# Gate, value and up projections as 2x2x2 block products by Strassen's seven, in an attention and mixture kernel on one NeuronCore

## The reference

```python
# attention: B, H, S, D = 4, 8, 576, 64, causal by blocks of 64 positions
scores = scale * (q @ k^T), -1e9 where block_i < block_j
attn   = softmax(scores);  x = (attn @ v) as 2304 tokens x 512
# gated layer: d_model 512, d_ff 1536
x = (sigmoid(x @ w_gate) * (x @ w_val)) @ w_out
# experts: E = 4, F = 1024, every token goes through every expert
p = domain_probs / (domain_probs.sum(-1) + 1e-9)
out = sum over e of p[:, e] * (relu(x @ w1[e]) @ w2[e])
```

## Time and profile before

| What | us |
|---|---|
| three runs | 1543.72, 1544.6, 1545.54 |
| median | 1544.6 |
| the profiled execution: its span, first to last instruction | 1543.3 |

### The profile page before, as it was taken

The page is one execution under the profiler, slowest core; times in us unless marked ns, Lnnn a source line. Parts: engine busy times, 40 slices in busy tenths (PEclk is TensorE's granted clock), DMA queues, the critical chain, the costliest instruction groups (busy, mean ns, idle before and its releaser), DMA issues.

```text
span 1543.3 us, 27668 instructions
## 1 busy us (share of the span) xinstructions
PE 1495.3 (97%) x8320; PEld 1376.8 (89%) x8320; DVE 663.8 (43%) x1309; ACT 578.4 (37%) x1267; POOL 160.5 (10%) x350
## 2 busy tenths in 40 slices
PE   6999998899999999999999999999999999999998
PEld 4777777899989999999999899999899999999997
DVE  4888888444222442425442333324344323323332
ACT  4777877555222222224541222222233312222221
POOL 3555555100000000001000000000010000000000
PEclk9999999999999999999999999999999999999999
DMA  7767674122222222213221212222232222222221
GB/s 174 176 163 168 163 176 113 50 67 62 67 58 68 68 56 68 66 56 104 61 75 55 62 55 70 67 68 54 59 107 66 62 61 70 63 61 68 57 65 55
DMA packets 196061, 126.71 MB, mean 82 GB/s; under 512 B 65792, under 2 KB 170272, under 8 KB 196000
## 3 DMA queue, kind: packets, MB, share of 16 engines
q1 hardware_dynamic: 194496, 121.15, 29.5%
q0 software_dynamic: 1504, 4.76, 0.9%
HBM read 92.84 MB, written 4.72 MB: 63 GB/s over the span
## 4 chain that ended last, share of the span: by engine, by line
PE 89%; DVE 5%; issue 3%; ACT 2%; SPq 1%; DVEq 0%; DMA 0%; ACTq 0%; POOL 0%; POOLq 0%
PE pb L810 27%; PE pb L808 27%; PE pb L809 27%; PE pt L438 2%; PE ov L456 2%; PE st L470 1%; DVE ptl L368 1%; DVE nmax L347 1%; PE st L426 1%; PE st L427 1%; ACT probs L275 1%; DVE x L383 1%; DVE ktl L374 1%; DVE qtl L374 0%; ACT pth L297 0%
## 5 line engine op out<-in xcount | busy, mean ns | idle before, releaser
L808 PE MATMUL pb<-xh,wl 128*128 128x384 f32 x1344 | 451.1, 336 | 9.0 <-DVE xl L683 6.5
L810 PE MATMUL pb<-xh,wh 128*128 128x384 f32 x1344 | 450.9, 335 | 0.0
L809 PE MATMUL pb<-xl,wh 128*128 128x384 f32 x1344 | 450.3, 335 | 0.0
L715 DVE SCALAR_TENSOR_TENSOR rl<-pb,rh 128x384 fp32r<-128x384 f32 x192 | 107.1, 558 | 508.4 <-ACT rh L617 508.4
L617 ACT ACTIVATE rh<-pb 128x384 fp32r<-128x384 f32 x192 | 94.5, 492 | 584.1 <-PE pb L810 584.1
L808 PEld LDWEIGHTS pb<-xh,wl 128*128 128x128 f32 x1344 | 252.9, 188 | 14.7 <-ACT wh L601 5.6
L809 PEld LDWEIGHTS pb<-xl,wh 128*128 128x128 f32 x1344 | 252.7, 188 | 3.5
L810 PEld LDWEIGHTS pb<-xh,wh 128*128 128x128 f32 x1344 | 252.7, 188 | 0.0
L683 DVE TENSOR_TENSOR wl<-raw,wh 128x512 fp32r<-128x512 f32 x298 | 196.6, 690 | 125.0 <-ACT wh L601 118.6
L810 PE MATMUL pb<-wh,rh 128*128 128x512 f32 x576 | 226.0, 392 | 0.0
L809 PE MATMUL pb<-wl,rh 128*128 128x512 f32 x576 | 225.7, 392 | 0.0
(11 more groups left out here) (74 smaller groups left out, 1601.5 us busy)
## 6 DMA issues: line engine op xcount, KB each, us to landing
raw<-in_moe_w_dram SPq DMA_DIRECT2D x192, 256.0 KB, 2.8
raw<-in_moe_w_gate_dram SPq DMA_DIRECT2D x36, 256.0 KB, 2.9
raw<-in_moe_w_val_dram SPq DMA_DIRECT2D x36, 256.0 KB, 2.9
raw<-in_moe_w_out_dram SPq DMA_DIRECT2D x36, 256.0 KB, 2.9
qhl<-qth SPq DMA_DIRECT2D x32, 144.0 KB, 2.5
qhl<-qtl SPq DMA_DIRECT2D x32, 144.0 KB, 2.5
qlh<-qtl SPq DMA_DIRECT2D x32, 144.0 KB, 2.5
qlh<-qth SPq DMA_DIRECT2D x32, 144.0 KB, 2.7
```

The lines of the kernel that those rows point to most:

```text
L715: nc.vector.scalar_tensor_tensor(rl[:, f % 2, a * TILE:(a + 1) * TILE], pb[:, 6 + a, 0:TILE], 0.0, rh[:, f % 2, a * TILE:(a + 1) * TILE].b ...
L808: nc.tensor.matmul(acc, lhs[1], rhs[0], start=start, stop=False)
L809: nc.tensor.matmul(acc, lhs[0], rhs[1], start=False, stop=False)
L810: return nc.tensor.matmul(acc, lhs[0], rhs[0], start=False, stop=stop)
```

## The change

Products of the gate, the value and the up projections are no longer computed as they stand. A unit (`unit`) takes a block of weights of 512 inputs by 256 features and the 768 tokens, both cut into 2x2 blocks (256 inputs, 128 features, 384 tokens). Four sums of weight blocks (`sums_of_weights`, GpSimd) and four sums of token blocks (`x_dve_first`, `x_dve_rest`, VectorE, once for a layer and super tile) are formed, and TensorE does seven block products (Winograd's form), each of 2 chunks by 3 matmuls of 384 columns: 42 matmuls in place of 48. P1, P6, P7 and P4 of a unit add up in one PSUM bank (a), P5 and P3 in a second (b), P2 has a third (c). What stands in bank a after P1 and after P6, and in bank b after P5, is copied out by ScalarE (`copy_of`, into s1b, u2b and s5b) before the next product is added on top of it, and VectorE adds the copy to another bank to get a block of the result (`c11`, `c12`, `c22`); the fourth block is bank a after P4.

Units of a super tile: 12 of the gated layer (gate and value in turn) and 4 for each of the 4 experts; there are 84 in all. While unit n multiplies, the engines split the seven weight blocks of unit n + 1 (`hi_a`, `hi_s`, `hi_4`, `lo_a`, `lo_s`, `lo_4`) and finish unit n - 1. `us` (the sums of weight blocks) has one buffer; `ura`, `uh`, `ul` have two. The first unit of the gated layer and of each expert is a head: there is nothing before it to interleave, and ScalarE does the copies of banks a and b before the next weights. P4 of a unit runs in the next unit, between P5 and P6. `down` follows after all four units of an expert, with its own pieces (`craw`, `ch`, `cl`); relu's split works on 3 blocks at once (1152 columns) and on the fourth alone; the hidden value's on 4 (1536 columns).

Everything is unrolled; there are no hardware loops. The attention's result goes through DRAM (`x1d`), a batch at a time. `tail_act` and `tail_dve` put the splits of unit 0's weights and all splits and sums of the first super tile's tokens into the attention's last 17 steps, the last ones ahead of the output of heads 30 and 31 in each queue. TensorE begins the gated layer after the last head's output. Output rows are sent from SP's queue as they are done, in place of GpSimd's. `mixed` is not cleared; expert 0 writes it.

The core of the diff; the first `unit` is TensorE's, the second ScalarE's, the third VectorE's, and `k` in `tail_act` counts the steps past the last score (attention's steps keep their order; their loop over bodies is written out):

```diff
-            over_model_dims(2 * v + a, 2 * u + v, a).then_inc((done, w_used)[a], 1)
+            def product(n, j, x, start, stop):
...
+                r, w, b = n % 2, W_OF[j], X_OF[j]
+                for c in range(2):
+                    mm = three(bank(n, x), (uh[r][:, w, c, :], ul[r][:, w, c, :]), (xch[:, b, c, :], xcl[:, b, c, :]),
+                               start and c == 0, stop and c == 1)
+                mm.then_inc(pd[j], 1)
...
+            def p4(n):
+                blocks(n, 4)
+                pe.wait_ge(w4_lo, n + 1)
+                pe.wait_ge(c22_ok, n + 1)
+                product(n, 4, "a", False, True)
+            def unit(n):
...
+                product(n, 1, "a", True, False)
+                pe.wait_ge(ws_lo, n + 1)
...
+                product(n, 5, "b", True, False)
+                if not head:
+                    p4(n - 1)
+                    p6(n)
...
+                product(n, 2, "c", True, True)
+                if head:
+                    p6(n)
...
+                pe.wait_ge(s5_ok, n + 1)
+                product(n, 3, "b", False, True)
...
+                pe.wait_ge(u2_ok, n + 1)
+                product(n, 7, "a", False, False)
...
+            def p6(n):
+                blocks(n, 6)
+                pe.wait_ge(s1_ok, n + 1)
+                product(n, 6, "a", False, False)
...
+            def unit(n):
+                if more and before:
+                    hi_a(act, n + 1)
+                    hi_s(act, n + 1)
+                copy_of(n, "a", s1b, 1, c11_ok, s1_ok)
+                copy_of(n, "b", s5b, 5, c22_ok, s5_ok)
+                if more and not before:
+                    hi_a(act, n + 1)
+                    hi_s(act, n + 1)
+                if before:
+                    c21(n - 1)
+                if more:
+                    hi_4(act, n + 1)
+                if before and kind(n - 1) == "val":
+                    hidden_hi(n - 1)
+                copy_of(n, "a", u2b, 6, c12_ok, u2_ok)
+                if before:
+                    rest(n - 1)
...
+            def unit(n):
+                if before:
+                    c22(n - 1)
+                    if kind(n - 1) == "val":
+                        gated_rest(n - 1)
+                if more:
+                    lo_a(dve, n + 1)
+                    lo_s(dve, n + 1)
+                if before and kind(n - 1) == "val":
+                    gated_21(n - 1)
+                if before and kind(n - 1) == "up":
+                    r21(n - 1)
+                if more:
+                    lo_4(dve, n + 1)
+                if before and kind(n - 1) == "val":
+                    hidden_lo(n - 1)
+                c11(n)
+                c12(n)
+                if before and kind(n - 1) == "up":
+                    r_rest(n - 1)
...
+        def hi_s(act, n):
+            act.wait_ge(us_ok, 4 * n + 4)
+            if n >= 2:
+                act.wait_ge(pd[7], n - 1)
...
+        def sums_of_weights(pool, n):
...
+            pool.wait_ge(u_in[r], 32 * (n // 2 + 1))
+            if n:
+                pool.wait_ge(ws_lo, n)
+            pool.sem_inc(pool_on, 1)
+            nc.gpsimd.tensor_tensor(us[:, 0, :], a21, a22, ALU.add).then_inc(us_ok, 1)
+            nc.gpsimd.tensor_tensor(us[:, 2, :], a11, a21, ALU.subtract).then_inc(us_ok, 1)
+            pool.wait_ge(us_ok, 4 * n + 1)
+            nc.gpsimd.tensor_tensor(us[:, 1, :], us[:, 0, :], a11, ALU.subtract).then_inc(us_ok, 1)
+            pool.wait_ge(us_ok, 4 * n + 3)
+            nc.gpsimd.tensor_tensor(us[:, 3, :], a12, us[:, 1, :], ALU.subtract).then_inc(us_ok, 1)
...
+        def tail_act(act, k, qk_ps):
+            if k == 0:
+                hi_a(act, 0)
+            if k == 1:
+                hi_s(act, 0)
+            if k == 2:
+                hi_4(act, 0)
+                act.wait_ge(qk_ps, STEPS)
+                act.wait_ge(xb_in, 16)
+            if k in (3, 4):
+                x_act_first(act, 0, k - 3)
+            if k in (6, 9):
+                x_act_b21(act, 0, k // 3 - 2)
+            if k in (7, 10):
+                x_act_rest(act, 0, k // 3 - 2)
```

1261 lines of the change are left out of this document (718 added, 543 removed).

## The result

| Kernel | median us (4 runs) | lowest and highest | profiled span |
|---|---|---|---|
| before, on the same chip | 1545.01 | 1543.72 to 1545.54 | 1543.3 (the profile read above) |
| changed | 1493.93 | 1492.58 to 1496.96 | 1490.8 |

The ratio is 0.9674 (95% interval 0.966 to 0.9688): faster by 51.1 us, 3.3%.

The account below looks back on a forecast made before the run. The prediction took TensorE's matmul stream as the bound. Its terms, -87.3 + 31 + 13 + 18 - 8 + 13 - 3 = -23.3, gave 1520 us against the profiled 1543.3, with a range of 1494 to 1548.

Parts of the forecast that it names:

- The removed matmuls: TensorE's block products: 84 units with 6 matmuls less each, 504 x 0.1733, forecast at -87.3 us.
- The fourth rival: TensorE gets no relief: seven products of 42 matmuls run at the old 8.3 us a unit; chance 0.02.
- (e): The attention's tail: added splits delay TensorE's start of the gated layer from 279.6 to 292.6, +13 us (7 to 16).
- (g): Terms put at nothing: the transfers, including x1 out and back, and the unrolled loops.
- (f): The kernel's end: SP's output issues run beside the additions, forecast at -3 us.
- (a): Second unit of each of 15 phases: P6 waits 1.85 us for s1b behind GpSimd's sums; +31 us in all.
- (b): The copy u2b late for P7: +0.3 at 15 heads, +0.6 at 15 gate units, together +13 with rounding.
- (c): VectorE's c22 late before P4, by 0.5 us at some 35 places if VectorE and GpSimd exclude each other: +18.
- (d): TensorE's earlier waits of 9.0 us: 8 go because the blocks' splits come piecewise, -8 us.
- the first rival: VectorE and GpSimd don't hinder each other: (a) and (c) shrink, 19 us less, 1501 us; chance 0.2.
- The second rival: GpSimd's ring of sums becomes the bound: +42, 1562 us at 0.914 a sum; chance 0.25 for GpSimd more loaded than priced.
- The third rival: ScalarE's and VectorE's waits fall into slack, so (a) to (c) halve: 1489 us; chance 0.08.

## Why the prediction was right or wrong

**The removed matmuls** brought -87.4 us for -87.3. The fourth rival (no relief for TensorE) is refuted by that line.

**(e) The tail**, +13 for +13.3, **agrees because of terms that cancel, and that is luck.** The 13.3 us are three things. Writing out the attention's loop took away 6.4 up to the last scores (265.28 to 258.84), which (g) had put at nothing. The changed kernel's own attention gave back 4.2 (258.84 to 263.05), where the one large difference in the traces is the wait for q behind x1's transfer; (g) had named just this, "costs several us if a stack of q or k queues behind it", and put it at nothing as well. The tail itself, from the last scores to the stage's first matmul, went from 14.3 to 29.9: 15.5 us, within the 7 to 16 that (e) allowed and 2.5 over its 13. Part of that excess is the step "I put 3 us on that", ScalarE's wait for the first four sums: it was 3.91 there and, through VectorE's queue, 6.14 on TensorE. A sum that agrees doesn't show that its terms do. (Its own terms, 265.28 + 7.8 + 12.4 + 3 + 3.9, give 292.4 and not the 292.6 that stands there.)

**(f) The end**, -3.1 for -3.

**(a) The second units: place, releaser and chain are right, the size is not.** 17.3 us for 31 (19.0 with the matmul behind each). Of 1.85 us at a place 1.13 were measured. The hand-over to TensorE was 0.06 and not 0.45 (0.39 less). The sums were done at 8.98 and not 9.6 (0.62 less): VectorE held them up, but by 0.33 at the last sum only. And P6 was due 0.24 earlier than I had it, because the wait for the head's `u2b` did not come. 1.85 - 0.39 - 0.62 + 0.24 is 1.08, near the 1.13. The first experts of the super tiles cost 1.18, 0.05 more than the others, where I had put 1 more.

**(b) u2b and (c) c22: again the places are right and the size is not.** With (d) they are +7.4 for +23. c22 was late at 39 places, where I had some 35, by 0.23 on the mean and not by 0.5: 8.9 us, 11.9 with the matmul behind each, for 18. `u2b` was late at the 15 gate units, by 0.18 and not by 0.6, and at 3 heads of the 15: 3.9, or 5.7 with the matmul behind, for 13. In the head, ScalarE ends `u2b` at 506.91, 4.95 after the head's start, when P7 is due at 5.2: with 0.45 it is late by 0.2, with 0.06 to 0.15 it is in time. In a gate unit behind a value unit I had TensorE starting P7 at 6.8, with P7 due at 6.24. The timeline of ScalarE and of TensorE there:

```profile
344.51 1.49 ACT L816 ACTIVATE hh<-cb 128x1536 fp32r<-128x1536 f32 x1 [0.72 <-DVE cb L937]
345.90 0.47 ACT L786 ACTIVATE u2b<-pb 128x384 f32<-128x384 f32 x1
```

```profile
346.43 0.44 PE L1056 MATMUL pb<-xch,ul 128*128 128x384 f32 x1
```

The split starts where I had it (4.4 into the unit); `u2b` ends at 346.37, TensorE starts 0.06 later, and P7 was due at 346.29: 0.14 late where 0.6 was forecast. Besides the hand-over I had left out the 0.1 by which the two ScalarE operations overlap. For c22 the dearest gaps are five of 0.63 to 0.81, three of them at the end of the gated layers; here TensorE starts 0.15 us after VectorE has ended:

```profile
380.75 0.41 PE L1056 MATMUL pb<-xch,ul 128*128 128x384 f32 x1 [0.64 <-DVE cb L925]
```

At the other 34 places c22 is late by 0.11 to 0.21.

**The step that failed is the size of the waits in (a), (b) and (c), through one price and one choice.** The price: 0.45 us for a hand-over to TensorE, from one place of a looped program. In the changed kernel it is 0.06 after ScalarE and 0.15 after VectorE. The working charges it at the 15 second units and the 15 gate units, where it is 0.39 too dear; for c22 the working doesn't show it, but 0.3 on top of the measured 0.23 is the 0.5 that stood there. By my estimate from these rows that is 15 x 0.39 + 15 x 0.39 + 39 x 0.3 = 23 of the 29 us. The kernel with the loops out shows that the price falls, not what each wait would cost at the old one. The choice: exclusion of the two engines at "some 2 us a unit". They do exclude each other, so the first rival (no hindrance) is refuted as a mechanism, although its 1501 lay nearer to the result; but the lengthening is (779 - 690) + (658 - 420), 0.33 us a unit, and 0.27 more in 18 gated units, and lies mostly where VectorE has slack. Removing it gave 5.3 us, where 19 was the forecast's difference. The two errors add up to more than 29; against them stand the matmul behind each late one (75 places, 6.7 us), which the sum had not at all, and the 3.6 by which P6 was due earlier.

**The second rival** (GpSimd's ring): the ring is real, and a fifth sum of 0.74 us cost 34 us. It did not decide because the unhindered sum came at 0.743, 3% over the estimate. Its point of decision was too near as well: five sums are as long as four of 0.93, and with them the kernel was still 1% faster than before, though the gain was to be gone at 0.83. (Its own terms put that point at 0.87: four sums, 1.05, 1.22, 0.4 and 1.4 against 7.28 + 23.3/84.)

**The third rival** ("(a) to (c) halve", 1489) has the number nearest to what came, and it had a chance of 0.08. I had held against it that the waits of (a) follow from the order. They do; their length didn't, and it hung on a price read at one place. But its reason, that the waits fall into slack, is not what the trace shows for (a) and (c): the waits stand where the forecast had them, 15 and 39 places (35 in the forecast), and each is shorter on the mean. Of (b), the waits at 12 of the 15 heads did fall away.

## What to carry to other kernels

When many waits share one hand-over price, that price decides the sum: read it at several places, in code of the same kind (loops or straight), and put its own lower bound into the range. A term that is put at nothing needs a row too: here two of them, -6.4 and +4.2, were hidden in a line that agreed. A buffer that makes one engine wait for another may also keep two that exclude each other apart: free it only where the wait is late. When work goes into a tail, follow the queue for what it stands ahead of, and above all for an instruction that waits for a third engine.

## What the runs showed of the hardware

- A hand-over from VectorE to TensorE takes 0.45 us in the looped kernel; at the same place it is 0.10 with the loops written out, and in the changed kernel 0.06 (after ScalarE) and 0.15 (after VectorE, at 39 places). Written out, the attention's 160 steps were 6.4 us shorter with the same matmuls and element operations, and ScalarE loaded its activation tables 2 times in place of 25.
- A matmul of 384 columns behind one that came late starts 0.25 to 0.28 us after it, in a stream 0.1733.
- With a transfer of 1536 KB issued just ahead of them from the same queue, transfers of 144 KB took 6.1 to 6.9 us to land, without it 2.6 to 3.0.
- GpSimd's sums and VectorE's operations on two SBUF operands exclude each other: 779 and 658 ns beside sums, 690 and 419 beside clears or nothing, up to 1.71 for a sum of 0.73. Clears by GpSimd hinder nobody (741 ns each, VectorE unhindered).
- GpSimd's sum of two 128x256 blocks in float32 takes 743 ns, a clear of 128x768 takes 741.
- In the 20 us from 280.00 on, the granted clock was 0.66 of full speed in the changed kernel (0.91 before), and after TensorE's pause up to 292.91 its first matmuls start about 0.32 apart, the lower of its two levels (1.2 GHz), to about 296. From the windows of the changed kernel (columns as in the earlier trace rows):

```profile
280.00:300.00 20.00, 12.33 (x58) 11.89 (x59) 14.42 (x33) 10.27 (x22) 0.00 (x0) 0.66 0.28 86
```
